# Layer 2 of a fused attention and two-layer kernel: four blocks of 384 tokens instead of three of 512

## What is computed

```
x: 1536 tokens x 512, the output of layer 1
h = x @ w_in                      # 512 -> 2048
g = where(h >= 1, h, where(h <= -1, 0, (h + 1)**2 / 4))
out = g @ w_out                   # 2048 -> 512, float32
```

## Time and profile before

| | us |
|---|---|
| median of 2 runs | 649.15 |
| the two runs | 647.33, 650.98 |
| profiled execution, first to last instruction | 649.1 |

### The profile page before, as it was taken

The page is one execution under the profiler, slowest core; times in us unless marked ns, Lnnn a source line. Parts: engine busy times, 40 slices in busy tenths (PEclk is TensorE's granted clock), DMA queues, the critical chain, the costliest instruction groups (busy, mean ns, idle before and its releaser), DMA issues.

```text
span 649.1 us, 9400 instructions
## 1 busy us (share of the span) xinstructions
PE 627.6 (97%) x3144; PEld 510.9 (79%) x3144; DVE 356.3 (55%) x553; ACT 323.3 (50%) x622; POOL 30.4 (5%) x33
## 2 busy tenths in 40 slices
PE   5779989999999999999999999999999999999997
PEld 2648868888888888888888888888888888888885
DVE  6855455544455555445333447666666666666664
ACT  1844576773468686434333344444444444444442
POOL 3310000100010101000000000000000000000000
PEclk9989979999999999999999999999999999999999
DMA  9997936512922221322332223232253332333221
GB/s 282 261 308 215 223 98 149 160 54 99 253 97 70 75 88 57 97 98 97 97 97 97 65 66 97 97 97 97 97 164 97 97 97 97 125 134 97 97 81 65
DMA packets 49780, 78.51 MB, mean 121 GB/s; under 512 B 16481, under 2 KB 21601, under 8 KB 49505
## 3 DMA queue, kind: packets, MB, share of 16 engines
q1 hardware_dynamic: 49760, 78.27, 39.8%
HBM read 72.48 MB, written 3.15 MB: 117 GB/s over the span
## 4 chain that ended last, share of the span: by engine, by line
PE 88%; SPq 5%; DMA 3%; DVE 1%; ACT 1%; issue 1%; DVEq 0%; ACTq 0%
PE bank L409 49%; PE bank L472 20%; PE bank L454 14%; DMA v_tok<-v_rows_dram 2%; PE bank L344 2%; PE bank L335 2%; SPq L207 2%; DMA win_raw<-w_dram 1%; SPq L203 1%; PE bank L328 1%; PE bank L321 1%; SPq L226 1%; DVE k_sum L681 1%; SPq L233 0%; ACT prob L536 0%
## 5 line engine op out<-in xcount | busy, mean ns | idle before, releaser
L409 PE MATMUL bank<-x_hi,win_hi 128*128 128x512 f32 (+1 forms) x480 | 191.6, 399 | 0.0
L409 PE MATMUL bank<-x_lo,win_hi 128*128 128x512 f32 (+1 forms) x480 | 188.1, 392 | 0.0
L409 PE MATMUL bank<-x_hi,win_lo 128*128 128x512 f32 (+1 forms) x480 | 187.8, 391 | 0.0
L593 ACT ACTIVATE hid_hi<-v_tok 128x512 fp32r<-128x512 f32 x84 | 53.0, 631 | 128.4 <-DVE v_tok L804 75.5
L409 PEld LDWEIGHTS bank<-x_lo,win_hi 128*128 128x128 f32 x480 | 90.7, 189 | 19.4
L409 PEld LDWEIGHTS bank<-x_hi,win_hi 128*128 128x128 f32 x480 | 90.7, 189 | 19.2 <-issue 0.2
L409 PEld LDWEIGHTS bank<-x_hi,win_lo 128*128 128x128 f32 x480 | 90.7, 189 | 18.3 <-issue 0.2
L774 DVE TENSOR_TENSOR hid_lo<-v_tok,hid_hi 128x512 fp32r<-128x512 f32 x84 | 65.5, 780 | 56.1 <-ACT hid_hi L593 56.0
L764 DVE TENSOR_TENSOR win_lo<-win_raw,win_hi 128x512 fp32r<-128x512 f32 (+1 forms) x84 | 76.9, 916 | 19.5 <-ACT win_hi L569 19.5
L472 PE MATMUL bank<-wout_hi,hid_hi 128*128 128x512 f32 x192 | 74.8, 389 | 0.3 <-ACT hid_hi L593 0.3
L472 PE MATMUL bank<-wout_hi,hid_lo 128*128 128x512 f32 x192 | 74.8, 390 | 0.0
(11 more groups left out here) (54 smaller groups left out, 576.4 us busy)
## 6 DMA issues: line engine op xcount, KB each, us to landing
wout_raw<-w_dram SPq DMA_DIRECT2D x84, 256.0 KB, 2.6
win_raw<-w_dram SPq DMA_DIRECT2D x36, 512.0 KB, 4.1
win_raw<-w_dram SPq DMA_DIRECT2D x48, 256.0 KB, 3.0
k_slot<-k_t_dram SPq DMA_DIRECT2D x24, 192.0 KB, 4.7
v_slot<-v_rows_dram SPq DMA_DIRECT2D x24, 192.0 KB, 5.2
v_tok<-v_rows_dram SPq DMA_DIRECT2D x4, 768.0 KB, 8.9
out_dram<-v_slot SPq DMA_DIRECT2D x12, 256.0 KB, 3.0
k_raw<-k_t_dram SPq DMA_DIRECT2D x2, 1056.0 KB, 12.1
```

The source lines that it names most:

```text
L409: last = nc.tensor.matmul(dst[:], a, m, start=k == 0 and i == 0, stop=k == KD - 1 and i == 2)
L593: nc.scalar.activation(hid_hi[:, r], hid[:, r], ACT.Copy).then_inc(hid_hi_ready, 1)
```

## The change

`TB2` = 384, `NBLK2` = 4 and `J2` = 3 take the place of `TB`, `NBLK` and `KD` = 4 in layer 2. Its steps are 4 x 16 = 64 instead of 48. A projection streams 384 columns. An output part has 3 groups of 128 tokens. The elementwise operations on hidden values are 384 wide in 512-wide buffers. At the end of a block ScalarE copies banks 0 and 2, VectorE bank 1, and the last bank's copy is ScalarE's. Weights are loaded and split once for each step, as before. Layer 1 keeps its blocks of 512. The first `out2` of layer 2 waits for all copies out of layer 1's accumulators ahead of its first bank, where before each bank waited for its own copy.

```
+TB2 = 384
+NBLK2 = TOK // TB2
+J2 = TB2 // P
 N1 = NBLK * CH1
-N2 = NBLK * CH2
+N2 = NBLK2 * CH2
...
-            def project(dst, r, c0, tok):
+            def project(dst, r, c0, tok, n=TB):
...
-                    x = (x_hi[:, k, bass.ds(tok, TB)], x_lo[:, k, bass.ds(tok, TB)])
+                    x = (x_hi[:, k, bass.ds(tok, n)], x_lo[:, k, bass.ds(tok, n)])
                     for i, (a, m) in enumerate(passes(w, x)):
-                        last = nc.tensor.matmul(dst[:], a, m, start=k == 0 and i == 0,
+                        last = nc.tensor.matmul(dst[:, 0:n], a, m, start=k == 0 and i == 0,
...
             def out2(n, r, free=None, ends=False):
...
-                for j in range(KD):
+                for j in range(J2):
...
-            for k in range(NBLK):
+            for k in range(NBLK2):
                 n0 = N1 + k * CH2
-                into_hidden2(n0 + 1, 1, k * TB)
-                out2(n0, 0, free=[((y_act_ready, y_dve_ready)[j % 2], 2 * (k - 1) + j // 2 + 1) if k else
-                                  (acc_read, KD * NBLK + j + 1) for j in range(KD)])
+                into_hidden2(n0 + 1, 1, k * TB2)
+                out2(n0, 0, free=[((y_act_ready, y_dve_ready)[j % 2], (2 - j % 2) * (k - 1) + j // 2 + 1) if k else
+                                  (acc_read, KD * (NBLK + 1)) for j in range(J2)])
...
             def layer2_even(k):
 
                 if k:
-                    act.wait_ge(stored, 16 * KD * k)
-                for j in range(0, KD, 2):
-                    act.wait_ge(acc_done, (KD - 1) * (NBLK + k) + j + 1)
+                    act.wait_ge(stored, 16 * J2 * k)
+                for j in range(0, J2, 2):
+                    if j < J2 - 1:
+                        act.wait_ge(acc_done, (KD - 1) * NBLK + (J2 - 1) * k + j + 1)
+                    else:
+                        act.wait_ge(out_done, N1 + (k + 1) * CH2)
                     nc.scalar.activation(y_out[:, j], acc_ps[j][:], ACT.Copy).then_inc(y_act_ready, 1)
...
             def layer2_odd(k):
...
-                for j in range(1, KD, 2):
-                    if j < KD - 1:
-                        dve.wait_ge(acc_done, (KD - 1) * (NBLK + k) + j + 1)
-                    else:
-                        dve.wait_ge(out_done, N1 + (k + 1) * CH2)
+                for j in range(1, J2, 2):
+                    dve.wait_ge(acc_done, (KD - 1) * NBLK + (J2 - 1) * k + j + 1)
                     nc.vector.tensor_copy(y_out[:, j], acc_ps[j][:]).then_inc(y_dve_ready, 1)
```

More of the change, by code:

```diff
@@ L277, in store @@
             def store(k):
-                for j in range(KD):
-                    sp.wait_ge((y_act_ready, y_dve_ready)[j % 2], 2 * k + j // 2 + 1)
-                    sp.dma_start(out[k * TB + j * P:k * TB + (j + 1) * P, :], y_out[:, j]).then_inc(stored, 16)
+                for j in range(J2):
+                    sp.wait_ge((y_act_ready, y_dve_ready)[j % 2], (2 - j % 2) * k + j // 2 + 1)
+                    sp.dma_start(out[k * TB2 + j * P:k * TB2 + (j + 1) * P, :], y_out[:, j]).then_inc(stored, 16)
             def load_chunks(k, start, stop):
@@ L307, in _ @@
                         load_w(2 * i + (n0 + r), w2[2 * i + r], IN2, r)
-            store(NBLK - 1)
-            sp.wait_ge(stored, 16 * NBLK * KD)
+            store(NBLK2 - 1)
+            sp.wait_ge(stored, 16 * NBLK2 * J2)
         @block.tensor
@@ L473, in out2 @@
                                                 stop=ends and i == 2)
-                    if ends and j < KD - 1:
+                    if ends and j < J2 - 1:
                         last.then_inc(acc_done, 1)
@@ L513, in _ @@
             out1(n0 + CH1 - 1, 1, ends=True)
-            for k in range(NBLK):
+            for k in range(NBLK2):
                 n0 = N1 + k * CH2
-                into_hidden2(n0 + 1, 1, k * TB)
-                out2(n0, 0, free=[((y_act_ready, y_dve_ready)[j % 2], 2 * (k - 1) + j // 2 + 1) if k else
-                                  (acc_read, KD * NBLK + j + 1) for j in range(KD)])
+                into_hidden2(n0 + 1, 1, k * TB2)
+                out2(n0, 0, free=[((y_act_ready, y_dve_ready)[j % 2], (2 - j % 2) * (k - 1) + j // 2 + 1) if k else
+                                  (acc_read, KD * (NBLK + 1)) for j in range(J2)])
                 with pe.Fori(1, CH2 // 2) as i:
                     for r in range(2):
-                        into_hidden2(2 * i + (n0 + r), r, k * TB)
+                        into_hidden2(2 * i + (n0 + r), r, k * TB2)
                         out2(2 * i + (n0 + r - 1), 1 - r)
-                if k < NBLK - 1:
-                    into_hidden2(n0 + CH2, 0, (k + 1) * TB)
+                if k < NBLK2 - 1:
+                    into_hidden2(n0 + CH2, 0, (k + 1) * TB2)
                 out2(n0 + CH2 - 1, 1, ends=True)
@@ L589, in gate, with hidden_hi @@
                 nc.scalar.activation(act1[:, r], ps[:], ACT.Silu).then_inc(act1_ready, 1)
-            def hidden_hi(n, r):
+            def hidden_hi(n, r, t=TB):
                 act.wait_ge(hid_ready, n + 1)
-                nc.scalar.activation(hid_hi[:, r], hid[:, r], ACT.Copy).then_inc(hid_hi_ready, 1)
+                nc.scalar.activation(hid_hi[:, r, 0:t], hid[:, r, 0:t], ACT.Copy).then_inc(hid_hi_ready, 1)
             def step1(n, m, r, next_cols):
@@ L603, in step2 @@
                 act.wait_ge(in_done, n + 1)
-                nc.scalar.activation(act1[:, r], in_ps[r][:], ACT.Relu, scale=0.5, bias=half[:, 0:1]
+                nc.scalar.activation(act1[:, r, 0:TB2], in_ps[r][:, 0:TB2], ACT.Relu, scale=0.5, bias=half[:, 0:1]
                                      ).then_inc(act1_ready, 1)
-                hidden_hi(n, r)
+                hidden_hi(n, r, TB2)
             def layer1_hi(k):
@@ L667, in _ @@
                     step2(2 * i + n0, i + n0 // 2, 0)
-                step2(n0 + CH2 - 1, n0 // 2 + CH2 // 2 - 1, 1, IN2 if k < NBLK - 1 else 0)
-            layer2_even(NBLK - 1)
+                step2(n0 + CH2 - 1, n0 // 2 + CH2 // 2 - 1, 1, IN2 if k < NBLK2 - 1 else 0)
+            layer2_even(NBLK2 - 1)
         @block.vector
@@ L770, in wout_rest, with hid_rest @@
                                         ).then_inc(wout_lo_ready, 1)
-            def hid_rest(n, r):
+            def hid_rest(n, r, t=TB):
                 dve.wait_ge(hid_hi_ready, n + 1)
-                nc.vector.tensor_tensor(hid_lo[:, r], hid[:, r], hid_hi[:, r], ALU.subtract
+                nc.vector.tensor_tensor(hid_lo[:, r, 0:t], hid[:, r, 0:t], hid_hi[:, r, 0:t], ALU.subtract
                                         ).then_inc(hid_lo_ready, 1)
@@ L800, in step2 @@
                 dve.wait_ge(hid_lo_ready, n - 1)
-                nc.vector.scalar_tensor_tensor(act2[:, r], act1[:, r], 1.0, act1[:, r], ALU.min, ALU.mult
+                a = act1[:, r, 0:TB2]
+                nc.vector.scalar_tensor_tensor(act2[:, r, 0:TB2], a, 1.0, a, ALU.min, ALU.mult
                                                ).then_inc(act2_ready, 1)
                 dve.wait_ge(act2_ready, c + 1)
-                nc.vector.tensor_tensor(hid[:, r], in_ps[r][:], act2[:, r], ALU.max).then_inc(hid_ready, 1)
-                hid_rest(n, r)
+                nc.vector.tensor_tensor(hid[:, r, 0:TB2], in_ps[r][:, 0:TB2], act2[:, r, 0:TB2], ALU.max
+                                        ).then_inc(hid_ready, 1)
+                hid_rest(n, r, TB2)
             def layer1_lo(k):
@@ L871, in _ @@
                     step2(2 * i + n0, 2 * i + k * CH2, 0)
-                step2(n0 + CH2 - 1, (k + 1) * CH2 - 1, 1, more=k < NBLK - 1)
-            layer2_odd(NBLK - 1)
+                step2(n0 + CH2 - 1, (k + 1) * CH2 - 1, 1, more=k < NBLK2 - 1)
+            layer2_odd(NBLK2 - 1)
         @block.gpsimd
```

4 lines of the change are left out of this document (2 added, 2 removed).

## The result

The changed kernel took 657.67 us (median of 657.29 and 658.06), the one before 649.15. The ratio of the runs is 1.0131, with a 95% interval from 1.0086 to 1.0177. It is slower by 1.3%: clear of no change, and less than the 2% that the prediction set as its line. The prediction was 652.5, with a range of 648 to 657: the direction held, the time lay 0.7 us above the range, and the loss is more than twice what the sum said.

What follows compares the result with a forecast made beforehand. The prediction took TensorE's matmul stream to bound layer 2. It summed 649.1 + 2.6 (matmuls) + 0.9 (entry) - 0.1 (end) = 652.5 us, with feeding and turns at 0, and a range of 648 to 657.

Steps and rivals of the forecast that it cites:

- The projection matmuls: Layer 2's matmul stream: 576 of 512 columns at 226.7 ns, 768 of 384 at 173.4 ns; +2.6 us.
- The bound: In layer 2 the matmul stream on TensorE alone sets the time; 48 steps, 261.1 of 649.1 us.
- A matmul of 384 columns: Layer 2 projections: 160.0 ns for columns plus a fixed 13.4 ns, 173.4 ns each; +2.6 us over 768.
- first rival: Layer 2 projections: remainder is proportional, 170.0 ns for 384 columns; 649.9 us in all, no change; chance 33%.
- The waits read before: Behind 380 us, TensorE waits for VectorE and ScalarE only three times, 0.3, 0.4 and 0.7 us, at the end.
- second rival: Layer 2 projections: weight loads of about 187 ns bind, pitch about 190 ns, 665.3 us, 2.5% slower; chance 8%.
- third rival: Layer 2 feeding: VectorE's 3.5 us exceed the 4.12 us step, or a load comes late; 655 to 662 us; chance 9%.
- the covers: Three turns between blocks: 0.9 us spare for bank copies, 2.0 us for the load behind the stores; cost 0.
- The entry: Start of layer 2: first output matmul waits for all four x_lo copies of layer 1; +0.9 us, bounds 0.4 and 1.5.
- The end: Last outputs: pause stays, last copy becomes ScalarE's, 0.594 instead of 0.683; -0.1 us, bounds -0.3 and +0.2.

Runs made afterwards that it cites:

- The narrow and the wide one-width runs: Changed kernel with all layer-2 matmuls at one width: output matmuls cut to 384 columns, 627.71 us; or projections streaming 512, 689.91 us.
- the 384-column run of the kernel before: Kernel before (three blocks, 48 steps) with layer-2 projections streaming only 384 of each block's 512 tokens; one run at 624.11 us.
- The 256-column run: Kernel before with layer-2 projections streaming only 256 of each block's 512 tokens; one run at 591.47 us.

## Why the prediction was wrong

The step that failed is the pricing of the matmuls, under "The projection matmuls": "The 576 cost 576 x 226.7 = 130.6 us", and 173.4 ns for each of the 768. It took a matmul's cost as a matter of its own width alone. The wide ones beside narrow ones cost 231 ns on average instead of 226.7, and the narrow ones 175.5 instead of 173.4. The first makes 64 x 41 ns = 2.6 us, the second 64 x 26 ns = 1.7: the larger part lies in the output matmuls, whose price the prediction took as known. That is 4.3 us, which no term of the sum and no rival held. The narrow and the wide one-width runs show it, and the 384-column run of the kernel before shows it without the four blocks.

It could have been seen. The trace of before has changes of width in layer 1, where scores and transposes of attention stand between projections. TensorE's timeline of the kernel before, right behind the eight short matmuls of the earlier trace rows:

```profile
124.25 0.39 PE L409 MATMUL bank<-x_hi,win_lo 128*128 x1
124.48 0.40 PE L409 MATMUL bank<-x_lo,win_hi 128*128 x1
124.71 0.40 PE L409 MATMUL bank<-x_hi,win_hi 128*128 x1
124.95 0.39 PE L409 MATMUL bank<-x_hi,win_lo 128*128 x1
125.17 0.39 PE L409 MATMUL bank<-x_lo,win_hi 128*128 x1
125.40 0.40 PE L409 MATMUL bank<-x_hi,win_hi 128*128 x1
```

These run 0.23, 0.23, 0.24, 0.22, 0.23. In nanoseconds the trace has 229 233 236 224 231 236 228 233 231 from 124.25 on, which are the numbers of the changed kernel's output part place by place. (The short ones are also of another format there, full fp32, so these rows alone would not have told which of the two it was.) I read these rows for the short matmuls and not for what follows them.

Point by point:

- **The bound.** Right. TensorE remains without a pause in layer 2 outside the entry and the end.
- **A matmul of 384 columns.** The settled 173.3 ns is what was taken, by the reason given: the remainder doesn't shrink with the width. The 256-column run confirms it. The first rival, the proportional price, falls.
- **The waits read before.** The 0.7 us that the prediction took as a wait of TensorE for the others is marked "issue" in the earlier trace rows, which names nobody; that changes nothing in the sum.
- **Weight loads** (second rival). Falls: it wanted 187 to 190 ns for each projection matmul, and they settle at 173.3. The 185 and 182 ns in the fourth and sixth place are not its sign, since the all-narrow run has 173 in every place.
- **The feeding** (third rival). Right to give it nothing. VectorE's turn takes 505.12 - 501.57 = 3.55 us where 3.5 was worked out, and the covers held at the turns. One of them was thinner than I said: the load behind the stores was issued 7.7 us behind the rectifier (7.8 forecast), but ScalarE had its weights only at 12.4 and not at 10.8. ScalarE's and VectorE's timelines at this turn, whose first rectifier is at 450.63:

```profile
463.07 0.63 ACT L559 ACTIVATE win_hi<-win_raw 128x512 fp32r<-128x512 f32 x1 [1.65 <-DMA win_raw<-w_dram]
...
463.73 0.69 DVE L757 TENSOR_TENSOR win_lo<-win_raw,win_hi 128x512 fp32r<-128x512 f32 x1 [1.72 <-ACT win_hi L559]
```

  `win_lo` is done at 464.42, and TensorE's next projection starts at 465.07: 0.65 us of cover were left, where the prediction had 2.0. This load, issued at 458.32, was there for ScalarE only 4.75 us later, and the prediction had taken the median of all loads, 3.0. That nothing was lost here owes something to luck.

- **The entry.** Right in place, cause and size: 0.9 us forecast, 0.9 measured, and 0.9 gained when it is taken out.
- **The end.** Forecast -0.1, and the account leaves nothing to it beyond 0.1 either way.
- **The total.** 3.4 us forecast for layer 2 against 7.7. The missing 4.3 are the disturbances.
- **The range.** Its upper end was 4.5 us over the forecast, made of scatter and a part of the feeding rival. The kernel before alone ran from 643.93 to 650.12 us in eleven runs on one chip, 3.1 us to either side, and from 645.06 to 652.95 on the other, where I took 1.8 from two runs. So the 0.7 us by which the time missed the range say little, and the changed kernel's median on another chip, 654.87, lies inside it. What shows the fault is the count from a mark: 7.7 us against 3.4.

**What stays open.** Why a change of width disturbs the next matmuls, and what sets the size: 67 ns for a step with two changes, 120 with eighteen, and another pattern at 256 columns. All runs changed widths only together with the bank written and the operands read. The one-width runs change bank and operands in the same places without any disturbance, so these alone are no cause, but the mechanism within TensorE was not found.

## What to carry to other kernels

In a stream of matmuls back to back, sum a fixed remainder for each matmul apart from its columns, and look at the distances behind a change of width, not only at the settled value: fewer matmuls of one width are cheaper for the same work. Three blocks of 512 gave both parts of the loop 512 columns, and losing that cost more (4.3 us) than the 192 extra matmuls (2.6 us). When a change touches one stage, count from a mark inside the program: that told 0.9 us, where timed runs of one kernel scatter by 6 to 8.

## What the runs showed of the hardware

- A settled fp32r matmul costs its columns at 2.4 GHz plus 13.3 ns: 120.0, 173.3 and 226.7 ns at 256, 384 and 512 columns, at a granted clock of 1.00. The Trainium skill ("TensorE: Matmul & The Clock Gate", Back-to-back issue gap) has plus 2.5 ns; these traces don't agree.
- After a change between 384 and 512 columns, six narrow matmuls carry 26 ns and nine wide ones 41 ns beyond that. In 61 steps of the changed kernel's profile each place stays within 2 ns of its median, but for the one where TensorE pauses at the end.
- Weight loads with a recorded duration of 188 to 192 ns follow each other every 120 ns beside the narrow matmuls of the 256-column run.
